# Last dense block: the last two F pieces taken by groups of 128 rows, each with its own signal, copy and store

## The chip, the cores and the metric

One core of a Trainium2 chip. The time of a kernel is the device time of one execution in microseconds (us); of several runs the median is given. The engines named below are PE (TensorE: the matmul stream, and PEld its weight loads), DVE (VectorE), ACT (ScalarE), POOL (GpSimd) and SP (SyncE, which here only issues DMAs). "L412" is line 412 of the kernel.

## What is computed

The program chains an attention-like recurrence, a routed mixture of experts, and a dense layer pair. Only the last part matters here; it works on x of 3072 rows and 384 columns:

```
def _moe2_ref(x, w_in, w_out):          # w_in 384 x 2048, w_out 2048 x 384
    h = x @ w_in
    relu6 = np.clip(h + 3.0, 0.0, 6.0)
    g = h * relu6 / 6.0
    return (g @ w_out).astype(np.float32)
```

Each product in fp32 is made of three matmuls in a faster format: every operand is split into a high and a low part, and hi·hi, hi·lo and lo·hi are added up in PSUM.

## The kernel before

**Tiling.** The dense part takes the 3072 rows in NBLK = 6 blocks of BLK = 512 rows. F2 = 2048 is cut into G2 = 16 pieces of 128. For each block and piece f, PE makes the piece of h, transposed (9 matmuls of 512 columns into one bank: 3 chunks of 128 of the 384 columns, 3 matmuls each); ACT makes `cut` from it (L692), DVE makes `g` (L1248), ACT rounds it to `g_hi` (L695), and DVE forms the rest `g_lo` (L1250), all on tiles of 128 x 512. The `g` tiles have F on the partitions and the 512 rows of the block along the free axis. Then the function `second` (L935) multiplies that piece by w_out: for each of the BT = 4 groups t of 128 rows, three matmuls of 384 columns (function `three`, L868 to L871) whose weights are the 128 columns t of `g_hi` and `g_lo`. They add into four banks `p_O[0..3]`, one for each group, which the trace calls bank_YT, bank_L, bank_P and bank_X. The first of the 16 pieces starts a bank's sum and the last ends it.

**Order on PE.** It is written out by hand in `blocks`. Piece f of h is followed by `second` of piece f - 2, so that the elementwise chain of a piece has time. After the loop over f come `second` of piece 14 and `second` of piece 15. In every block but the last, the next block's first pieces of h follow directly.

**The end of a block.** `second` of each piece adds 1 to the semaphore `s_O`. When it has counted all 16 pieces, ACT copies banks 0 and 1 to `o_sb` (L707) and adds 1 to `s_oA` after the second copy; DVE copies banks 2 and 3 (L1260) and adds 1 to `s_oV`. SP waits for `s_oA` and stores the first 256 rows (384 KB), then waits for `s_oV` and stores the other 256 rows (L410). The stores add 16 to `s_out[0]` and `s_out[1]`. At the very end SP waits for both (L417). The copies of a block wait for the stores of the block before, since `o_sb` has one buffer.

**Loops.** `dense_loop` writes blocks 0 and 1 out, runs blocks 2 and 3 as a hardware loop, and writes out blocks 4 and 5. Only block 5 has `last=True`. The input of block 5 is transposed during block 4, so SP has nothing but the two stores to do in block 5.

Of the kernel before, what the change touches and what calls it, by code (L numbers as in the profile page):

```python
# [9 lines left out]
ACT = mybir.ActivationFunctionType  # L10
AXX = mybir.AxisListType.X

P = 128
B, H, S, HD = 4, 8, 768, 48
D = H * HD
# [9 lines left out]
G2 = F2 // P  # L25
# [7 lines left out]
BLK = 512  # L33
NBLK = N // BLK
BT = BLK // P
# [2 lines left out]
TINY = 1e-9  # L38

ROUND = (4, 8, 12)  # L40
SHIFT = 4
RT_SHIFTED, RT_CHOICE, RT_SUMS, RT_TOTAL, RT_PICKED, RT_ALL = 3, 7, 8, 12, 13, 18
C_W1, C_W2 = (1, 2, 3), (1, 2, 3, 4)
# [27 lines left out]
def chained_moe_program(nc, r, k, v, w, u, w_skip, w_gate, w1, w2, w_in, w_out, out, x_dram, slot_dram):  # L71
    ctx = ExitStack()
    with ctx:
# [36 lines left out]
        p_mT, p_H, p_O = bank[0], bank[1:4], bank[4:8]  # L110
# [50 lines left out]
        wo_hi = sb("wo_hi", [P, G2, D], F32R)  # L161
# [13 lines left out]
        wo_lo = sb("wo_lo", [P, G2, D], F32R)  # L175
# [7 lines left out]
        class Region:  # L183
# [61 lines left out]
        g_hi = [de(f"g_hi{i}", [P, BLK], F32R) for i in range(4)]  # L245
        g_lo = [de(f"g_lo{i}", [P, BLK], F32R) for i in range(4)]
        o_sb = de("o_sb", [P, BT, D])
# [23 lines left out]
        s_m, s_mT, s_mhi, s_mlo, s_H, s_cut, s_g, s_ghi, s_glo, s_O, s_oA, s_oV = (  # L271
            sem(x) for x in ("s_m", "s_mT", "s_mhi", "s_mlo", "s_H", "s_cut", "s_g", "s_ghi", "s_glo", "s_O", "s_oA", "s_oV"))
        s_out = [sem(f"s_out{half}") for half in range(2)]
# [42 lines left out]
        def _(eng):  # L316
# [82 lines left out]
            def load_m(blk):  # L399
                eng.dma_start(m_in[:, :, :], x_dram[bass.ds(blk * BLK, BLK), :].rearrange("(t p) n -> p t n", p=P)).then_inc(s_m, 16)  # L400

            def blocks(blk, i, first=False, last=False):
                if not last:
                    if not first:
                        eng.wait_ge(s_mT, KC * blk + KC)
                    load_m(blk + 1)
                for half, done in enumerate((s_oA, s_oV)):
                    eng.wait_ge(done, blk + 2)
                    ts = slice(half * BT // 2, (half + 1) * BT // 2)
                    eng.dma_start(out[bass.ds(blk * BLK + half * (BLK // 2), BLK // 2), :].rearrange("(t p) n -> p t n", p=P),  # L410
                                  o_sb[:, ts, :]).then_inc(s_out[half], 16)
# [2 lines left out]
                eng.sem_inc(done, 16)  # L414
            dense_loop(eng, blocks)
            for done in s_out:
                eng.wait_ge(done, 16 * (NBLK + 1))  # L417


        @block.gpsimd  # L420
# [141 lines left out]
        def _(eng):  # L562
# [82 lines left out]
            def win_hi(f):  # L645

                piece = slice(f * P, (f + 1) * P)
                eng.activation(wi_hi[:, :, piece], wi_raw[:, :, piece], ACT.Copy).then_inc(s_wihi, 1)
# [37 lines left out]
            def blocks(blk, i, first=False, last=False):  # L686
                for f in range(G2):
                    t = G2 * blk + f
                    eng.wait_ge(s_H, t + 1)

                    eng.wait_ge(s_g, t + SHIFT - 1)
                    eng.activation(cut[f % 2][:, :], p_H[f % 3][:, :], ACT.Relu, bias=0.5, scale=1.0 / 6.0).then_inc(s_cut, 1)  # L692
                    eng.wait_ge(s_g, t + SHIFT + 1)
                    eng.wait_ge(s_O, t + SHIFT - 3)
                    eng.activation(g_hi[f % 4][:, :], g[f % 2][:, :], ACT.Copy).then_inc(s_ghi, 1)  # L695
                    if not last and f in ROUND:
                        rows_hi(1 - i, ROUND.index(f), KC * (blk + 1) + ROUND.index(f))
                    if first:
                        if f == 0:
                            eng.wait_ge(s_wo, 16 * W_PARTS)  # L700
                        wout_hi(f)
                        if f + HI_FIRST < G2:
                            win_hi(f + HI_FIRST)
                eng.wait_ge(s_O, G2 * (blk + 1) + SHIFT)
                eng.wait_ge(s_out[0], 16 * blk + 16)
                for t in range(BT // 2):
                    a = eng.activation(o_sb[:, t, :], p_O[t][:, 0:D], ACT.Copy)  # L707
                a.then_inc(s_oA, 1)
# [14 lines left out]
        def _(eng):  # L723
# [5 lines left out]
            for q in range(NPAIR):  # L729
                last = eng.transpose(p_X[:, q * P:(q + 1) * P], u_less[:, q:q + 1].to_broadcast([P, P]), ident[:, :])  # L730
            last.then_inc(s_uT, 1)
            eng.wait_ge(s_tab, TAB_K)
            for q in range(NPAIR):
                last = eng.transpose(p_kT[:, q * P:(q + 1) * P], powT_k[:, q, :], ident[:, :])
# [133 lines left out]
            def three(dst, a_hi, a_lo, b_hi, b_lo, start, stop):  # L868
                eng.matmul(dst, a_hi, b_hi, start=start, stop=False)  # L869
                eng.matmul(dst, a_hi, b_lo, start=False, stop=False)  # L870
                return eng.matmul(dst, a_lo, b_hi, start=False, stop=stop)  # L871
# [57 lines left out]
            def rows_mT(kc, done):  # L929
# [2 lines left out]
                    a = eng.transpose(p_mT[:, t * P:(t + 1) * P], m_in[:, t, kc * P:(kc + 1) * P], ident[:, :])  # L932
                a.then_inc(s_mT, 1)

            def second(blk, f, first=False):  # L935
                t0 = G2 * blk + f
                eng.wait_ge(s_glo, t0 + 1)
                if first:
                    eng.wait_ge(s_wolo, f + 1)
                if f == 0:  # L940
                    eng.wait_ge(s_oA, blk + 1)
                    eng.wait_ge(s_oV, blk + 1)
                for t in range(BT):
                    tok = slice(t * P, (t + 1) * P)
                    a = three(p_O[t][:, 0:D], g_hi[f % 4][:, tok], g_lo[f % 4][:, tok], wo_hi[:, f, :], wo_lo[:, f, :],
                              f == 0, f == G2 - 1)
                a.then_inc(s_O, 1)

            def blocks(blk, i, first=False, last=False):
                if not first:  # L950
                    eng.wait_ge(s_mlo, KC * (blk + 1))
                for f in range(G2):

                    eng.wait_ge(s_g, G2 * blk + (f - 1 if f < 2 else f - 2) + SHIFT)
                    if first:
                        eng.wait_ge(s_wilo, f + 1)
                    for kc in range(KC):
                        if first and f == 0:
                            eng.wait_ge(s_mlo, kc + 1)
                        piece = slice(f * P, (f + 1) * P)  # L960
                        a = three(p_H[f % 3][:, :], wi_hi[:, kc, piece], wi_lo[:, kc, piece],
                                  mT_hi[i][:, kc, :], mT_lo[i][:, kc, :], kc == 0, kc == KC - 1)
                    a.then_inc(s_H, 1)
                    if not last and f in ROUND:
                        kc = ROUND.index(f)
                        if kc == 0:
                            eng.wait_ge(s_m, 16 * (blk + 1))
                        rows_mT(kc, KC * (blk + 1) + kc)
                    if f >= 2:
                        second(blk, f - 2, first)  # L970
                second(blk, G2 - 2, first)
                second(blk, G2 - 1, first)

# [2 lines left out]
            for kc in range(KC):  # L976
                for t in range(TH):
                    for gain, done in ((gain_hi, s_gain_hi), (gain_lo, s_gain_lo)):
                        eng.wait_ge(done, t + 1)
                        a = eng.matmul(p_first_mT[kc], gain[t][:, kc * P:(kc + 1) * P], goes_to[t][:, :], start=False,  # L980
                                       stop=gain is gain_lo and t == TH - 1, skip_group_check=True)
# [5 lines left out]
        def _(eng):  # L987
            done = [0]
# [171 lines left out]
            last = NC - 1  # L1160
# [25 lines left out]
            def win_lo(f):  # L1186

                piece = slice(f * P, (f + 1) * P)
                eng.wait_ge(s_wihi, f + 1)
                eng.tensor_tensor(wi_lo[:, :, piece], wi_raw[:, :, piece], wi_hi[:, :, piece].bitcast(F32), ALU.subtract).then_inc(s_wilo, 1)  # L1190
# [52 lines left out]
            def blocks(blk, i, first=False, last=False):  # L1243
                for f in range(G2):
                    t = G2 * blk + f
                    eng.wait_ge(s_cut, t + 1)

                    eng.scalar_tensor_tensor(g[f % 2][:, :], cut[f % 2][:, :], 1.0, p_H[f % 3][:, :], ALU.min, ALU.mult).then_inc(s_g, 1)  # L1248
                    eng.wait_ge(s_ghi, t + 1)
                    eng.tensor_tensor(g_lo[f % 4][:, :], g[f % 2][:, :], g_hi[f % 4][:, :].bitcast(F32), ALU.subtract).then_inc(s_glo, 1)  # L1250
                    if not last and f in ROUND:
                        rows_lo(1 - i, ROUND.index(f), KC * (blk + 1) + ROUND.index(f))
                    if first:
                        wout_lo(f)
                        if f + LO_FIRST < G2:
                            win_lo(f + LO_FIRST)
                eng.wait_ge(s_O, G2 * (blk + 1) + SHIFT)
                eng.wait_ge(s_out[1], 16 * blk + 16)
                for t in range(BT // 2, BT):
                    a = eng.tensor_copy(o_sb[:, t, :], p_O[t][:, 0:D])  # L1260
                a.then_inc(s_oV, 1)
# [37 lines left out]
```

## Time and profile before

| | us |
|---|---|
| median of 3 runs (743.0 to 743.84) | 743.3 |
| the profiled execution, its own time | 737.41 |
| its span in the trace | 735.6 |
| PE busy in the span | 700.2 (95%) |
| end of the last matmul in the trace | 730.7 |

The span is what the instructions cover. The profiled execution's own time is 1.8 us longer than its span, and 5.9 us shorter than the median of the plain runs; differences within the trace are carried over to the median as they are. Matmul ends in the trace are modelled and overlap; the distance between the starts of two neighbours is the time that one takes in a stream.

### The profile page before, as it was taken

Reading aid. Unit: us, or ns where it says so; the run is one execution under the profiler, and the core shown is the slowest. Engines: PE = TensorE matmul, PEld = TensorE weight load, DVE = VectorE, ACT = ScalarE, POOL = GpSimd, SP = SyncE. Lnnn points to the kernel's source line nnn. Section 1 sums busy time; section 2 is a strip of 40 time slices with the busy share of each in tenths; the row PEclk is TensorE's granted clock in tenths of the full one; section 3 lists DMA queues with packets and bytes.
Section 4 is the critical chain, followed back from the end, with each engine's and each line's share of the span. In section 5 each row is a group of like instructions: output and inputs, shape, how many; then the busy total and the mean of one; then the engine's idle time right before and its main releaser. Section 6 shows DMA issues by size and latency. Waiting matters only on the chain.

```text
span 735.6 us, 13594 instructions
## 1 busy us (share of the span) xinstructions
PE 700.2 (95%) x5103; PEld 639.5 (87%) x5103; DVE 383.7 (52%) x767; ACT 324.3 (44%) x703; POOL 141.0 (19%) x189
## 2 busy tenths in 40 slices
PE   5999999929899999989999999999999999999997
PEld 3888888819899999979899899899999999998896
DVE  5576667566678888656544333433333333333332
ACT  3767767625555555635343232333233233223232
POOL 8648866450222222100000000000000000000000
PEclk9999999968999999999999999999999999999999
DMA  9788886114946666810002000200200020001001
GB/s 156 145 185 176 194 173 133 55 40 155 382 145 212 210 219 214 267 60 1 1 1 86 1 1 1 86 1 1 63 24 1 1 86 1 1 1 43 1 1 43
DMA packets 106986, 65.57 MB, mean 89 GB/s; under 512 B 79938, under 2 KB 102756, under 8 KB 106928
## 3 DMA queue, kind: packets, MB, share of 16 engines
q1 hardware_dynamic: 102864, 60.18, 30.6%
q0 software_dynamic: 2816, 4.60, 2.0%
q8 instruction: 37, 0.61, 0.3%
q10 hardware_dynamic: 1248, 0.02, 0.1%
q14 instruction: 21, 0.17, 0.1%
HBM read 53.69 MB, written 12.80 MB: 90 GB/s over the span
## 4 chain that ended last, share of the span: by engine, by line
PE 90%; DVE 2%; DMA 2%; ACT 2%; issue 2%; POOL 1%; POOLq 0%; DVEq 0%; SPq 0%; ACTq 0%
PE bank_A L870 8%; PE bank_A L871 8%; PE bank_A L869 8%; PE bank_A L807 4%; PE bank_L L869 4%; PE bank_L L871 4%; PE bank_L L870 4%; PE bank_P L871 4%; PE bank_P L870 4%; PE bank_P L869 4%; PE bank_kT L870 3%; PE bank_kT L871 3%; PE bank_kT L869 3%; PE bank_YT L871 3%; PE bank_YT L870 3%; PE bank_YT L869 3%
## 5 line engine op out<-in xcount | busy, mean ns | idle before, releaser
L1250 DVE TENSOR_TENSOR g_lo<-g,g_hi 128x512 fp32r<-128x512 f32 x96 | 66.5, 692 | 67.0 <-ACT g_hi L695 67.0
L695 ACT ACTIVATE g_hi<-g 128x512 fp32r<-128x512 f32 x96 | 60.7, 632 | 73.1 <-DVE g L1248 73.1
L1248 DVE SCALAR_TENSOR_TENSOR g<-cut,bank_A 128x512 f32<-128x512 f32 x60 | 41.2, 687 | 92.8 <-ACT cut L692 92.8
L692 ACT ACTIVATE cut<-bank_A 128x512 f32<-128x512 f32 x60 | 35.9, 598 | 101.3 <-PE bank_A L871 100.8
L871 PE MATMUL bank_A<-mT_hi,wi_lo 128*128 128x512 f32 x180 | 71.0, 394 | 0.0
L870 PE MATMUL bank_A<-mT_lo,wi_hi 128*128 128x512 f32 x180 | 70.9, 394 | 0.0
L869 PE MATMUL bank_A<-mT_hi,wi_hi 128*128 128x512 f32 x180 | 70.0, 389 | 0.0
L590 ACT ACTIVATE bank_A<-ident,own 128x128 f32<-128x128 f32 x192 | 59.1, 359 | 5.5 <-DVE A_sb L1041 3.0
L1248 DVE SCALAR_TENSOR_TENSOR g<-cut,bank_kT 128x512 f32<-128x512 f32 x36 | 24.7, 687 | 66.6 <-ACT cut L692 66.6
L692 ACT ACTIVATE cut<-bank_kT 128x512 f32<-128x512 f32 x36 | 21.5, 598 | 69.7 <-PE bank_kT L871 69.7
L674 ACT ACTIVATE hT_hi<-bank_A 128x256 fp32r<-128x256 f32 x48 | 18.4, 384 | 56.9 <-PE bank_A L871 56.9
L869 PE MATMUL bank_A<-xgT_hi,w_hi 128*128 128x256 f32 x144 | 41.6, 289 | 1.3 <-DVE xgT_lo L1207 1.3
L871 PE MATMUL bank_kT<-mT_hi,wi_lo 128*128 128x512 f32 x108 | 42.7, 396 | 0.0
L870 PE MATMUL bank_kT<-mT_lo,wi_hi 128*128 128x512 f32 x108 | 42.6, 395 | 0.0
L869 PE MATMUL bank_kT<-mT_hi,wi_hi 128*128 128x512 f32 x108 | 42.1, 390 | 0.1
L871 PE MATMUL bank_A<-xgT_hi,w_lo 128*128 128x256 f32 x144 | 41.5, 288 | 0.0
L870 PE MATMUL bank_A<-xgT_lo,w_hi 128*128 128x256 f32 x144 | 41.5, 288 | 0.0
L871 PEld LDWEIGHTS bank_A<-mT_hi,wi_lo 128*128 128x128 f32 x180 | 33.8, 188 | 7.2
L1041 DVE TENSOR_TENSOR A_sb<-bank_A,upto 128x512 f32<-128x512 f32 x48 | 30.9, 686 | 17.4 <-PE bank_A L807 17.2
L870 PEld LDWEIGHTS bank_A<-mT_lo,wi_hi 128*128 128x128 f32 x180 | 33.7, 187 | 6.0
L869 PEld LDWEIGHTS bank_A<-mT_hi,wi_hi 128*128 128x128 f32 x180 | 33.8, 188 | 5.7
L1218 DVE TENSOR_TENSOR w_lo<-raw,w_hi 128x384 fp32r<-128x384 f32 x64 | 35.9, 561 | 0.0
(240 smaller groups left out, 1848.3 us busy)
## 6 DMA issues: line engine op xcount, KB each, us to landing
raw<-in_moe_w_dram SPq DMA_DIRECT2D x24, 512.0 KB, 5.8
raw<-in_moe_w_dram SPq DMA_DIRECT2D x7, 1536.0 KB, 6.9
r_in<-in_r_dram SPq DMA_DIRECT2D x24, 192.0 KB, 4.4
k_in<-in_k_dram SPq DMA_DIRECT2D x24, 192.0 KB, 4.7
v_in<-in_v_dram SPq DMA_DIRECT2D x24, 192.0 KB, 3.4
x_scratch<-y_sb SPq DMA_DIRECT2D x24, 192.0 KB, 2.3
out_dram<-o_sb SPq DMA_DIRECT2D x12, 384.0 KB, 2.8
m_in<-x_scratch SPq DMA_DIRECT2D x5, 768.0 KB, 5.3
```

The costliest lines, as they stand in the source:

```text
L590: a = eng.activation(p_A[:, o, q * P:(q + 1) * P], ident[:, :], ACT.Copy, scale=own[n % 2][:, 2 * q + o:2 * q + o + 1])
L674: eng.activation(hT_hi[:, f, :], p_h[f % 3][:, 0:TT], ACT.Relu).then_inc(s_hhi, 1)
L692: eng.activation(cut[f % 2][:, :], p_H[f % 3][:, :], ACT.Relu, bias=0.5, scale=1.0 / 6.0).then_inc(s_cut, 1)
L695: eng.activation(g_hi[f % 4][:, :], g[f % 2][:, :], ACT.Copy).then_inc(s_ghi, 1)
L807: m = eng.matmul(p_A[:, o, q * P:(q + 1) * P], kT[i][half, q, :], rT[i][half, q, :], start=False, stop=True, skip_group_check=True)
L869: eng.matmul(dst, a_hi, b_hi, start=start, stop=False)
L870: eng.matmul(dst, a_hi, b_lo, start=False, stop=False)
L871: return eng.matmul(dst, a_lo, b_hi, start=False, stop=stop)
L1041: eng.tensor_tensor(A_sb[i][:, o, :, :], p_A[:, o, :].rearrange("s (q t) -> s q t", q=NPAIR), mask, ALU.mult).then_inc(s_Aev, 1)
L1218: eng.tensor_tensor(w2_lo[:, f, :], raw2[:, f, :], w2_hi[:, f, :].bitcast(F32), ALU.subtract).then_inc(s_w2lo, 1)
L1248: eng.scalar_tensor_tensor(g[f % 2][:, :], cut[f % 2][:, :], 1.0, p_H[f % 3][:, :], ALU.min, ALU.mult).then_inc(s_g, 1)
L1250: eng.tensor_tensor(g_lo[f % 4][:, :], g[f % 2][:, :], g_hi[f % 4][:, :].bitcast(F32), ALU.subtract).then_inc(s_glo, 1)
```

## The change

In the last block only, the order on PE after the loop over f is turned inside out: for each group t in the order 0, 2, 1, 3 first the three matmuls of piece 14 and then the three of piece 15, and then a signal. Each group is copied as soon as its signal is there, ACT taking groups 0 and 1 and DVE groups 2 and 3, each copy with its own count, and SP stores each group of 128 rows (192 KB) by itself, in the same order. The final wait counts two stores more in all, one for each of the two semaphores. In all blocks ACT and DVE now wait for the store of the block before ahead of the wait for `s_O`, and not behind it.

```
+LAST_ROWS = (0, 2, 1, 3)
...
 SP:
+                if last:
+                    for t in LAST_ROWS:
+                        half = t // (BT // 2)
+                        eng.wait_ge((s_oA, s_oV)[half], blk + 2 + t % (BT // 2))
+                        eng.dma_start(out[blk * BLK + t * P:blk * BLK + (t + 1) * P, :], o_sb[:, t, :]).then_inc(s_out[half], 16)
+                    return
...
-                eng.wait_ge(done, 16 * (NBLK + 1))
+                eng.wait_ge(done, 16 * (NBLK + BT // 2))
...
 ACT:
+                eng.wait_ge(s_out[0], 16 * blk + 16)
+                if last:
+                    for t in range(BT // 2):
+                        eng.wait_ge(s_O, G2 * blk + G2 - 2 + SHIFT + LAST_ROWS.index(t) + 1)
+                        eng.activation(o_sb[:, t, :], p_O[t][:, 0:D], ACT.Copy).then_inc(s_oA, 1)
+                    return
                 eng.wait_ge(s_O, G2 * (blk + 1) + SHIFT)
-                eng.wait_ge(s_out[0], 16 * blk + 16)
...
 PE:
+            def product(t, f):
+
+                tok = slice(t * P, (t + 1) * P)
+                return three(p_O[t][:, 0:D], g_hi[f % 4][:, tok], g_lo[f % 4][:, tok], wo_hi[:, f, :], wo_lo[:, f, :],
+                             f == 0, f == G2 - 1)
...
                 for t in range(BT):
-                    tok = slice(t * P, (t + 1) * P)
-                    a = three(p_O[t][:, 0:D], g_hi[f % 4][:, tok], g_lo[f % 4][:, tok], wo_hi[:, f, :], wo_lo[:, f, :],
-                              f == 0, f == G2 - 1)
+                    a = product(t, f)
                 a.then_inc(s_O, 1)
...
+                if last:
+                    for t in LAST_ROWS:
+                        for f in (G2 - 2, G2 - 1):
+                            eng.wait_ge(s_glo, G2 * blk + f + 1)
+                            a = product(t, f)
+                        a.then_inc(s_O, 1)
+                    return
                 second(blk, G2 - 2, first)
                 second(blk, G2 - 1, first)
...
 DVE:
+                eng.wait_ge(s_out[1], 16 * blk + 16)
+                if last:
+                    for t in range(BT // 2, BT):
+                        eng.wait_ge(s_O, G2 * blk + G2 - 2 + SHIFT + LAST_ROWS.index(t) + 1)
+                        eng.tensor_copy(o_sb[:, t, :], p_O[t][:, 0:D]).then_inc(s_oV, 1)
+                    return
                 eng.wait_ge(s_O, G2 * (blk + 1) + SHIFT)
-                eng.wait_ge(s_out[1], 16 * blk + 16)
```

## Rows read from the trace of the kernel before

**Rows 1.** The page: PE busy and its clock in 40 slices; the chain by engine
```profile
PE   5999999929899999989999999999999999999997
...
PEclk9999999968999999999999999999999999999999
...
PE 90%; DVE 2%; DMA 2%; ACT 2%; issue 2%; POOL 1%; POOLq 0%; DVEq 0%; SPq 0%; ACTq 0%
```

**Rows 2.** Timeline, 730.3 to 736 us: start, duration, engine, line, what
```profile
730.36 0.34 PE L871 MATMUL bank_X<-wo_hi,g_lo 128*128 128x384 f32 x1
730.73 0.49 ACT L707 ACTIVATE o_sb<-bank_YT 128x384 f32<-128x384 f32 x1 [4.28 <-PE bank_X L871]
730.73 0.56 DVE L1260 COPY o_sb<-bank_P 128x384 f32<-128x384 f32 x1 [3.56 <-PE bank_X L871]
731.12 0.48 ACT L707 ACTIVATE o_sb<-bank_L 128x384 f32<-128x384 f32 x1
731.21 0.55 DVE L1260 COPY o_sb<-bank_X 128x384 f32<-128x384 f32 x1
731.63 0.89 SPq L410 DMA_DIRECT2D out_dram<-o_sb  x2
```

**Rows 3.** Stores and SP's waits at the end: duration ns min/median/max, landing counted from issue
```profile
L410 SPq DMA_DIRECT2D out_dram<-o_sb x2: 372/420/469, 731.6 to 732.0; - x2
...
DMA to landing us min/median/max: 2.5/2.8/3.1
...
SPq L417 <- DMA out_dram<-o_sb: 2.6, 1, 2.6
...
L73 SPq COMPARE_BRANCH  x1: 38/38/38, 735.2 to 735.2; - x1
```

**Rows 4.** Windows at the end: stretch, length, busy of PE, PEld, DVE, ACT, POOL, clock, DMA share, GB/s
```profile
731.63:732.52 0.89, 0.00 (x0) 0.00 (x0) 0.12 (x1) 0.00 (x0) 0.00 (x0) 1.00 0.01 2
732.52:734.70 2.18, 0.00 (x0) 0.00 (x0) 0.00 (x0) 0.00 (x0) 0.00 (x0) 1.00 1.01 359
734.70:735.60 0.90, 0.00 (x0) 0.00 (x0) 0.00 (x0) 0.00 (x0) 0.00 (x0) 0.82 0.01 3
```

**Rows 5.** Timeline, 726.2 to 728.5 us: `second` of piece 14 starts, g_lo of piece 15
```profile
726.37 0.33 PE L869 MATMUL bank_YT<-wo_hi,g_hi 128*128 128x384 f32 x1
726.48 0.69 DVE L1250 TENSOR_TENSOR g_lo<-g,g_hi 128x512 fp32r<-128x512 f32 x1 [0.70 <-ACT g_hi L695]
...
726.72 0.33 PE L871 MATMUL bank_YT<-wo_hi,g_lo 128*128 128x384 f32 x1
...
726.89 0.33 PE L869 MATMUL bank_L<-wo_hi,g_hi 128*128 128x384 f32 x1
...
728.45 0.33 PE L869 MATMUL bank_YT<-wo_hi,g_hi 128*128 128x384 f32 x1
```

**Rows 6.** Timeline, 322.5 to 326 us: a short wait of PE for DVE
```profile
323.63 0.69 DVE L1241 TENSOR_TENSOR mT_lo<-bank_X,mT_hi 128x512 fp32r<-128x512 f32 x1 [0.52 <-ACT mT_hi L684]
...
323.94 0.39 PE L871 MATMUL bank_kT<-mT_hi,wi_lo 128*128 128x512 f32 x1
...
324.38 0.19 PEld L869 LDWEIGHTS bank_kT<-mT_hi,wi_hi 128*128 128x128 f32 x1 [0.48 <-DVE mT_lo L1241]
324.38 0.50 PE L869 MATMUL bank_kT<-mT_hi,wi_hi 128*128 128x512 f32 x1
324.49 0.19 PEld L870 LDWEIGHTS bank_kT<-mT_lo,wi_hi 128*128 128x128 f32 x1
324.72 0.40 PE L870 MATMUL bank_kT<-mT_lo,wi_hi 128*128 128x512 f32 x1
```

**Rows 7.** The copies to o_sb in all six blocks: count, duration ns min/median/max
```profile
L1260 DVE COPY o_sb<-bank_P x6: 557/558/558, 391.4 to 730.7; 128x384 f32<-128x384 f32 x6
L1260 DVE COPY o_sb<-bank_X x6: 547/547/548, 391.9 to 731.2; 128x384 f32<-128x384 f32 x6
```

**Rows 8.** Stores of 192 KB in the first part: all 24; that of 150.3; that of 145.2
```profile
x_scratch<-y_sb SPq DMA_DIRECT2D x24, 192.0 KB, 2.3
...
L326 SPq DMA_DIRECT2D x_scratch<-y_sb x1: 320/320/320, 150.3 to 150.3; - x1
...
DMA to landing us min/median/max: 1.9/1.9/1.9
...
L326 SPq DMA_DIRECT2D x_scratch<-y_sb x1: 319/319/319, 145.2 to 145.2; - x1
...
DMA to landing us min/median/max: 2.5/2.5/2.5
```

**Rows 9.** Windows around PE's idle time ahead of the dense part
```profile
316.00:318.40 2.40, 0.06 (x2) 0.03 (x1) 2.34 (x5) 0.49 (x2) 0.97 (x1) 1.00 0.13 45
...
319.00:321.00 2.00, 2.00 (x6) 1.63 (x5) 0.36 (x2) 0.60 (x1) 0.00 (x0) 0.50 0.40 57
...
324.00:326.00 2.00, 1.95 (x9) 1.36 (x8) 1.26 (x3) 0.60 (x1) 0.00 (x0) 1.00 0.00 0
```

## The prediction, made before the changed kernel ran

> **What bounds the kernel now.** I read the page's slices first: PE is busy nine tenths of nearly every slice, falls in the very last one, and makes 90% of the chain of waits [rows 1]. The change touches nothing that PE does before 726 us, so the question is only how long the tail is behind the last matmuls. The timeline of the end comes next. The last matmul starts at 730.36; 0.37 later ACT and DVE both start copying, two banks each; ACT is done at 731.60, DVE at 731.76 [rows 2]. SP issues the first store at 731.63, right behind ACT, and the second at 732.05: the two issues fill 0.89 us to 732.52, and the second is the one of 0.47 [rows 2, 3]. The windows show data moving from 732.52 to 734.70 at 359 GB/s with all DMA engines busy: 0.79 MB cannot go faster [rows 4]. The stores land 2.5 and 3.1 us after their issue, so the last at 732.05 + 3.1 = 735.15, which agrees with SP's wait of 2.6 us from 732.52 on and its branch at 735.2; the span ends at 735.6, 0.45 later [rows 3]. From the last matmul's start to the end are thus 5.2 us, with nothing for PE to do. Two parts of them hang on the amount of work: the second copy of each engine, and 2.2 us of transfer, since all of the block's output starts at once.
>
> **The change part by part.**
>
> PE issues the same 24 matmuls of 384 columns. In a stream they are 0.174 us apart (726.37 to 728.45 for twelve) [rows 5]; six a group are 1.04 us. Only the order differs, with eight waits on `s_glo` where there were two. Now the three matmuls of group 0, piece 15, come fourth, in the slot of 726.89, and not at 728.45. They need `g_lo` of piece 15, which DVE ends at 726.48 + 0.69 = 727.17 [rows 5]. So **a new stall** appears that was hidden by nine matmuls of piece 14. Its price by the nearest event: mT_lo ended at 324.32, the weight load began at 324.38 (0.06 later) and the next load at 324.49, which is when the first matmul really entered (0.11); the matmul after it started at 324.72 against 323.94 + 2 x 0.23 = 324.40, a loss of 0.32, the same as 324.49 against 324.17 [rows 6]. Here that gives a load at 727.23, entry at 727.34, and a loss of 727.34 - 726.89 = **+0.45 us**. Bounds: at least 727.17 - 726.89 = 0.28; at most, were the whole load of 0.19 exposed, 727.42 - 726.89 = 0.53. Queued behind this wait are the 21 remaining matmuls; all move by 0.45. The other waits on `s_glo` are met by then: nothing. The last matmul starts at 730.81, not 730.36.
>
> Copies. By the same 0.37 behind a group's last matmul, groups 0, 2, 1 and 3 can be copied from 728.06, 729.10, 730.14 and 731.18. Each engine gets one every 2.1 us and needs 0.49 (ACT) or 0.56, so the first three lie beside PE's work. Would a copy be slower while PE writes other banks? In the five earlier blocks the copies ran beside PE and took 547 to 558 ns, as in the last [rows 7]. Behind PE remains one DVE copy of 0.55: done at 731.73. Only 0.03 is won on the old 731.76, since the stall eats nearly what the dropped copy gives.
>
> Stores. SP has two DMAs more, four of 0.32 to 0.47 each, about 1.04 apart, in the order in which the groups come; nothing waits behind them on SP, POOL issues nothing here. The third is issued near 730.66 and its 196 KB are through by 732.1. The fourth is issued at 731.76 (0.03 behind the copy, as before): 732.05 - 731.76 = **-0.29 us**, because it no longer stands behind a neighbour's issue. Its landing is the term that decides. In this profile 24 stores have just this form (128 partitions x 384 fp32 to DRAM): the median of 2.3 is taken among other traffic, the one at 150.3 on a quiet machine took 1.9 and the worst that I count as quiet (145.2) took 2.5 [rows 8]. The last store will be alone, so I take 1.95, nearest to the 1.9: landing at 733.71. Against 3.1 that is **-1.15 us**; at 2.5 it would be -0.6. The windows agree: 0.20 MB at 359 GB/s are 0.55 us, a quarter of the 2.2 that pass now.
>
> On the size of the DMA the Trainium skill speaks against the change: "DMA: Bandwidth & Descriptors", section "Rules for kernel authors", says to put small transfers together, and its anatomy section gives each DMA a fixed 2.0 us plus bytes over 436 GB/s, measured on the GpSimd path. By that 192 KB would take 2.45, an estimate from the page, and the gain would be 0.5 less; the 1.9 of [rows 8] says otherwise.
>
> The waits on `s_out` that moved ahead of `s_O` ask for stores issued a block (68 us) earlier: nothing, either way. The end of the program behind the last landing stays 0.45, with one wait more that is already met.
>
> **Sum.** -0.29 - 1.15 = -1.44 (the +0.45 of PE and the -0.48 of the dropped copy are both in the -0.29). The profiled execution would take 737.41 - 1.44 = 735.97. It stands 5.9 us under the median of the runs, and nothing in the tail suggests that the change touches that offset: 743.3 - 1.4 = **741.9**. With both bounds at their good ends (stall 0.28, landing 1.9) the gain is 1.66, at their bad ends (0.53, 2.5) 0.81: 741.6 to 742.5.
>
> A measurement of this kernel can tell about 0.2%, which is 1.49 us, from no change. The forecast lies just short of it.
>
> **The rivals.**
>
> *A slower landing.* The last store takes 2.3 to 2.5, as the median and the quiet bad case of [rows 8] do, because starting a transfer and confirming it in DRAM does not shrink. Gain 0.9 to 1.1: 742.3. For it: one of the quiet stores did so. Against: the store at 150.3. The page's fixed cost points the same way. Chance 0.22.
>
> *Slower: the clock falls in the stall.* PE idles for about 0.45 us in front of its last 21 matmuls. After 2.4 us of idle time the granted clock of this kernel fell from 1.00 to 0.50, that is from 2.4 to 1.2 GHz, and matmuls ran so for over 3 us [rows 9]. If the new stall did that, the busy 21 x 0.174 = 3.65 us would at most double: +3.65 - 1.44 = +2.2, 745.5. It decides once more than 1.44 / 0.174, about 8 matmuls, run at the lower level. Against: the comparable wait of 0.44 us was followed by a window at 1.00 [rows 6, 9]. Chance 0.03.
>
> *The change doesn't do what it says, because the stores don't overlap.* If each had to land before the next starts moving, four of 1.95 from 728.6 on would end at 736.4, +1.2. Against: the two stores now, issued 0.42 apart, land 1.0 apart and not 2.5 [rows 3]. Chance 0.01.
>
> *No stall, or hardly one,* because matmuls of piece 14 get through later than the trace's starts say. Gain 1.7 and more: 741.5. The wait in [rows 6] speaks against it. Chance 0.06.
>
> *Nothing measurable is won,* because some engine's end that I don't see holds the program open. The last chain is stores, and SP's wait ends it [rows 3]. Chance 0.04.
>
> **How the numbers follow.** The forecast (gain 1.2 to 1.6) has 0.64. Since 1.44 lies 0.05 short of the bound of 1.49 and medians scatter by some 0.3, I give it a little less than half on the faster side: 0.30, plus 0.05 from the case without a stall and some 0.04 from scatter in the slow landing, 0.39. Slower by over 0.2% needs the clock or the stores in series: 0.04. The rest, 0.57, is within 0.2%. The range reaches from the case without a stall, with scatter (741.3), over the slow landing with scatter (742.9).
>
> **What would show it.** In the timeline of after: a gap on PE's weight loads from 726.9 to 727.2, ended by DVE's g_lo; 24 matmuls still 0.174 apart behind it; last matmul start near 730.8; copies 1.04 apart; four stores, the last near 731.76 and alone; landing 1.9 to 2.0; the span near 734.2. A gap over 0.6, a landing over 2.4, a clock under 1.00 in 727 to 731, or copies queued behind each other would prove the step in question wrong.

## The result, and the profile after

Over 22 runs each the changed kernel has a median of 742.11 us against 743.85 before. The recorded ratio, taken over all the runs, is 0.9979, with a 95% interval from 0.9969 to 0.9989 (the two medians alone give 0.9977). On the 743.3 us of the forecast that is 741.7, a gain of 1.56 us (0.8 to 2.3), where 741.9 and 1.44 were forecast. The gain lies at the bound of 0.2% that the forecast drew, a trifle beyond it. The interval covers both sides, so the side on which it falls is chance. Two stray executions of the later runs, one of 1762.7 us and one of 2070.15, are in no ratio.

The profiled execution of the changed kernel took 740.89 us with a span of 739.1, **longer** than the 737.41 and 735.6 of before. Single executions of either kernel differ by that much (740.2 to 745.5 in these runs), and the difference lies far from the change: the first matmul of the dense part starts at 322.8 before and at 327.8 after, while from there to the first product of piece 14 in block 5 both take 403.6 us, as do all the runs below. So the two traces are compared from that last point on. **The tail**, from the start of that matmul (bank_YT, `g_hi`) to the end of the span, is 735.6 - 726.37 = 9.23 us before [rows 5] and 739.1 - 731.37 = 7.73 after: 1.50 less. Spans have one decimal, so a tail is good to 0.05 and a difference of two to 0.1.

The timeline of after, 731.3 to 737 us (start, duration, engine, line, what), with the lines that answer to [rows 5] first:

```profile
731.37 0.33 PE L881 MATMUL bank_YT<-wo_hi,g_hi 128*128 128x384 f32 x1
731.48 0.69 DVE L1273 TENSOR_TENSOR g_lo<-g,g_hi 128x512 fp32r<-128x512 f32 x1 [0.70 <-ACT g_hi L702]
...
732.23 0.19 PEld L881 LDWEIGHTS bank_YT<-wo_hi,g_hi 128*128 128x128 f32 x1 [0.49 <-DVE g_lo L1273]
732.23 0.45 PE L881 MATMUL bank_YT<-wo_hi,g_hi 128*128 128x384 f32 x1 [0.17 <-DVE g_lo L1273]
732.34 0.19 PEld L882 LDWEIGHTS bank_YT<-wo_lo,g_hi 128*128 128x128 f32 x1
732.51 0.34 PE L882 MATMUL bank_YT<-wo_lo,g_hi 128*128 128x384 f32 x1
...
733.13 0.49 ACT L715 ACTIVATE o_sb<-bank_YT 128x384 f32<-128x384 f32 x1 [1.68 <-PE bank_YT L883]
...
733.65 3.48 SPq L412 DMA_DIRECT2D out_dram<-o_sb  x4
...
735.83 0.34 PE L883 MATMUL bank_X<-wo_hi,g_lo 128*128 128x384 f32 x1
736.21 0.56 DVE L1284 COPY o_sb<-bank_X 128x384 f32<-128x384 f32 x1 [1.46 <-PE bank_X L883]
```

The fourth matmul now waits for DVE: `g_lo` ends at 732.17, the weight load starts 0.06 later, and the next load at 732.34, when the first matmul has entered. In an unbroken stream it would have entered at 731.37 + 3 x 0.174 = 731.89: a stall of 0.45. The trace prints 0.49 for the load engine, counted from the end of its last load, and 0.17 for PE, since it counts a matmul as busy for 0.33 us while the next enters after 0.17; neither is the loss. The last matmul starts 4.46 us into the tail and not 3.99 [rows 2, 5]. One copy, DVE's, is behind it in place of two on each engine, and ends at 736.77. The window over the 21 matmuls behind the stall (length, busy of PE, PEld, DVE, ACT, POOL, granted clock, DMA share, GB/s) shows the clock at 1.00:

```profile
732.34:736.00 3.66, 3.66 (x21) 3.51 (x21) 0.56 (x1) 0.98 (x2) 0.00 (x0) 1.00 0.25 90
```

The stores of after, which answer to [rows 3] (duration ns, then landing us from issue, min/median/max), and SP's waits in the tail:

```profile
L412 SPq DMA_DIRECT2D out_dram<-o_sb x4: 332/338/345, 733.6 to 736.8; - x4
...
DMA to landing us min/median/max: 1.8/1.9/1.9
...
SPq L424 <- DMA out_dram<-o_sb: 1.5, 1, 1.5
...
L424 SPq EVENT_SEMAPHORE  x1: 17/17/17, 738.7 to 738.7; - x1
```

The DMA view of the last 4.0 us of each kernel, in slices of 0.1 us (busy tenths of the DMA engines, then GB/s), before from 731.6 on and then after from 735.1 on:

```profile
DMA  0000000007899999999999999999997100000000
GB/s 0 0 0 0 0 0 0 0 0 261 307 399 353 323 353 384 384 399 338 400 338 399 338 399 338 399 338 399 338 399 246 31 0 0 0 0 0 0 0 0
```

```profile
DMA  0000068989600078989500000699996100000000
GB/s 0 0 0 0 0 246 323 430 323 415 215 16 0 0 276 323 415 323 415 200 16 0 0 0 0 215 338 399 338 399 246 31 0 0 0 0 0 0 0 0
```

Before, one unbroken stretch of 2.2 us; after, short bursts of some 0.6 us that never touch, three of the four in view. Two of them come behind the start of the last matmul (735.83), at 736.5 and 737.6, and only the last lies behind the last copy as well. Behind the last burst, in both, come the same eight empty slices until the end.

### The profile page after: what moved, and what is told of

It reads as the page before. It is cut to its first block, busy times and chain, and to the rows that moved or that the text cites. A ratio compares the mean times of both kernels' runs of the same rounds, so it can differ in the third digit from the quotient of the medians.

```text
span 739.1 us, 13596 instructions
## 1 busy us (share of the span) xinstructions
PE 699.9 (95%) x5103; PEld 638.1 (86%) x5103; DVE 385.5 (52%) x767; ACT 324.4 (44%) x703; POOL 141.2 (19%) x189
## 4 chain that ended last, share of the span: by engine, by line
PE 86%; ACT 4%; DVE 3%; issue 3%; DMA 2%; another core or an unknown queue 1%; POOL 1%; POOLq 0%; ACTq 0%; SPq 0%; DVEq 0%
PE bank_A L882 8%; PE bank_A L883 8%; PE bank_A L881 8%; PE bank_A L819 4%; PE bank_L L881 4%; PE bank_L L883 4%; PE bank_L L882 4%; PE bank_P L883 4%; PE bank_P L882 4%; PE bank_P L881 4%; PE bank_kT L882 3%; PE bank_kT L883 3%; PE bank_kT L881 3%; PE bank_YT L883 3%; PE bank_YT L881 3%; PE bank_YT L882 3%
## 5 line engine op out<-in xcount | busy, mean ns | idle before, releaser
L819 PE MATMUL bank_A<-rT,kT 64*128 64x128 f32 x384 | 28.8, 290 | 8.8 <-ACT bank_A L597 6.1
```

The lines of the kernel that those rows point to most:

```text
L819: m = eng.matmul(p_A[:, o, q * P:(q + 1) * P], kT[i][half, q, :], rT[i][half, q, :], start=False, stop=True, skip_group_check=True)
```

## The experiments

Whole-kernel times scatter by some 0.5% between executions, so ratios have intervals of about 0.15% and can't part kernels that differ by half a us. The tails can. Here are both kernels and all twelve runs, with the tail read from the same anchor, the first matmul of piece 14's products. Where group 2 comes first, that is one into bank_P. Where piece 15 comes first, the anchor is put 0.11 before the start of DVE's `g_lo`; in the others it lies 0.11 to 0.12 before it.

| kernel | tail, us | ratio to before, 95% interval |
|---|---|---|
| before | 9.23 | 1 |
| the change | 7.73 | 0.9979 (0.9969 to 0.9989) |
| the change again (a0) | 7.77 | 0.9978 (0.9966 to 0.9990) |
| the change a third time (c1) | 7.78 | 0.9976 (0.9960 to 0.9992) |
| order 14, then 15, rest as the change (a1) | 7.37 | 0.9970 (0.9956 to 0.9984) |
| groups in pairs (a2) | 7.27 | 0.9979 (0.9963 to 0.9995) |
| pairs, ending on ACT (b3) | 7.09 | 0.9975 (0.9959 to 0.9991) |
| the same again (c2) | 7.16 | 0.9973 (0.9955 to 0.9992) |
| the same, final waits swapped (c4) | 7.20 | profile only |
| the change's order alone (a3) | 9.76 | 1.0010 (0.9996 to 1.0023) |
| two stores of 384 KB (b1) | 8.26 | 0.9999 (0.9982 to 1.0015) |
| copies only at the end (b2) | 9.28 | 1.0005 (0.9987 to 1.0024) |
| piece 15 of group 0 first (b4) | 8.24 | 0.9996 (0.9981 to 1.0010) |
| only the waits for old stores moved (c3) | 9.30 | 1.0000 (0.9984 to 1.0017) |

The ratios are the recorded ones and not quotients of medians (for a2 the medians would give 0.9993). Where a tail is 1 us shorter (b1, b4) they show no gain, and don't exclude it either. The tail of before stems from one profile, with c3 as its nearest repeat; that of the change was taken three times.

**The change again.**

> The changed kernel again. Tail = from the start of the first matmul of piece 14's products in the last block (bank_YT<-wo_hi,g_hi) to the end of the span: 9.23 us before, 7.73 us in the one profile of after. Theory (the gain is the last store, 192 KB alone in place of two of 384 KB, issued 0.3 us earlier in spite of a PE stall of 0.45 us): tail 7.7 to 7.8, time 1.5 us under before. Rival (the time differs because the earlier stages of the program ran otherwise): tail changes from profile to profile by more than 0.2 us.

> The changed kernel a third time, as the neighbour of the version below on one chip. Theory: tail 7.7 to 7.8, ratio to before 0.998. Rival (the ratio was luck of runs that scatter by 0.5% for other reasons): ratio 0.999 to 1.001 with the tail still 1.5 us shorter.

Tails of 7.77 and 7.78, ratios of 0.9978 and 0.9976. With spans as far apart as 732.3, 737.7 and 739.1 us, the tail moved by 0.05 in all, so the rival, a tail that moves by over 0.2, falls. The mean of the three is 7.76, so the change takes 1.47 us off the tail.

**PE's order alone.** In ACT's and DVE's branches for the last block and on SP:

```
-                        eng.wait_ge(s_O, G2 * blk + G2 - 2 + SHIFT + LAST_ROWS.index(t) + 1)
+                        eng.wait_ge(s_O, G2 * blk + G2 - 2 + SHIFT + BT)
...
-                    for t in LAST_ROWS:
-                        half = t // (BT // 2)
+                    for half, done in enumerate((s_oA, s_oV)):
+                        eng.wait_ge(done, blk + 3)
...
```

> PE's order of the change (group by group, stall included) alone; both engines copy only after the last group, and two stores of 384 KB as before. Theory: only the stall is left of the change: tail 9.23 + 0.45 = 9.7, time 0.4 to 0.5 us over before. Rival (the inside-out order itself brings something, for instance shorter matmul distances): tail 9.2 or less.

The tail is 9.76, 0.53 over before, where 0.45 was expected. The last matmul starts at 737.37 - 732.94 = 4.43 and not 3.99, which is the stall; another 0.06 is a later start of the copies (below), and the rest is within the rounding. The group-by-group order by itself brings nothing and costs its stall.

**No stall: two other orders on PE.** First, piece 14 of all groups and then piece 15 of all, with the signals, copies and stores of the change:

```
-                    for t in LAST_ROWS:
-                        for f in (G2 - 2, G2 - 1):
-                            eng.wait_ge(s_glo, G2 * blk + f + 1)
-                            a = product(t, f)
-                        a.then_inc(s_O, 1)
+                    for t, f in [(t, G2 - 2) for t in LAST_ROWS] + [(t, G2 - 1) for t in LAST_ROWS]:
+                        eng.wait_ge(s_glo, G2 * blk + f + 1)
+                        a = product(t, f)
+                        if f == G2 - 1:
+                            a.then_inc(s_O, 1)
```

> PE takes pieces 14 and 15 in the old sense (all groups of 14, then all of 15, groups in the order 0, 2, 1, 3); signals, copies and stores by group as in the change. No wait for g_lo, so the last matmul starts 3.99 us into the tail and not 4.46; groups end 0.52 apart and not 1.04. Theory: the PE stall is worth 0.45 us and the last store still lands in 1.9 to 2.0: tail 7.3, time 0.4 us under after. Rival (the reordering is what makes the gain, since it spaces the stores 1 us apart): the four stores, each 0.55 us of transfer, 0.52 us apart, run into each other, the last lands in 2.3 to 2.5: tail 7.6 to 7.8, no better than after.

The tail is 7.37, 0.39 under the change. The last matmul starts 736.22 - 732.23 = 3.99 into it. Its timeline and stores (as above):

```profile
736.22 0.34 PE L883 MATMUL bank_X<-wo_hi,g_lo 128*128 128x384 f32 x1
736.59 0.56 DVE L1284 COPY o_sb<-bank_X 128x384 f32<-128x384 f32 x1 [0.42 <-PE bank_X L883]
```

```profile
L412 SPq DMA_DIRECT2D out_dram<-o_sb x4: 344/351/453, 735.6 to 737.2; - x4
DMA to landing us min/median/max: 1.9/1.9/2.0
```

The stores come 0.52 us apart and move for 0.55 each, yet the slowest lands in 2.0. Crowding costs 0.1 of the 0.47 that the missing stall gives; the reordering is not what makes the gain.

Second, the groups in pairs, so that six matmuls cover the wait and the last two groups still end 1.04 apart:

```
+                    for t, f in ((0, G2 - 2), (2, G2 - 2), (0, G2 - 1), (2, G2 - 1), (1, G2 - 2), (1, G2 - 1), (3, G2 - 2), (3, G2 - 1)):
```

> As the change, but PE takes piece 14 of groups 0 and 2, then piece 15 of both, then groups 1 and 3 one after the other. Piece 15 is first needed 6 x 0.174 = 1.04 us into the tail, 0.1 to 0.2 us later than g_lo is done (0.80). Theory: no stall, stores of the last two groups still 1.04 us apart: last matmul starts at 3.99, tail 7.27 to 7.3, time 0.4 to 0.5 us under after. Rival (the stall costs nothing at the end because the last store's landing is bounded otherwise): tail 7.7.

Tail 7.27, as expected, and in its waits from 733.6 us on no line of PE or PEld is left:

```profile
ACT o_sb L715 <- PE bank_YT L883: 1.7, 1, 1.7
DVE o_sb L1284 <- PE bank_P L883: 1.5, 1, 1.5
DVE o_sb L1284 <- PE bank_X L883: 1.5, 1, 1.5
ACT o_sb L715 <- PE bank_L L883: 1.0, 1, 1.0
ACT g_hi L702 <- DVE g L1271: 0.8, 1, 0.8
DVE g_lo L1273 <- ACT g_hi L702: 0.7, 1, 0.7
```

**A longer stall.** For group 0, piece 15 comes before piece 14 (the matmul that ends the bank's sum is then piece 14's):

```
-                        for f in (G2 - 2, G2 - 1):
+                        for f in (G2 - 1, G2 - 2) if t == 0 else (G2 - 2, G2 - 1):
```

> The change, but for group 0 PE takes piece 15 before piece 14, so that the wait for g_lo comes with the very first product and the stall grows by 3 matmuls: from 0.45 to 0.45 + 0.52 = 0.97 us. Theory (every us of stall moves the end by a us, clock stays at full speed): tail 7.73 + 0.52 = 8.25, granted clock 1.00. Rival (a stall of PE ahead of its last 24 matmuls brings the clock down to half): matmuls 0.35 us apart, tail over 9.

Timeline, and the window over the last 24 matmuls (length, busy of PE, PEld, DVE, ACT, POOL, granted clock, DMA share, GB/s):

```profile
728.29 0.34 PE L883 MATMUL bank_X<-wo_hi,g_lo 128*128 128x384 f32 x1
728.57 0.69 DVE L1273 TENSOR_TENSOR g_lo<-g,g_hi 128x512 fp32r<-128x512 f32 x1 [0.70 <-ACT g_hi L702]
729.32 0.19 PEld L881 LDWEIGHTS bank_YT<-wo_hi,g_hi 128*128 128x128 f32 x1 [1.01 <-DVE g_lo L1273]
729.32 0.44 PE L881 MATMUL bank_YT<-wo_hi,g_hi 128*128 128x384 f32 x1 [0.69 <-DVE g_lo L1273]
...
729.60 0.34 PE L882 MATMUL bank_YT<-wo_lo,g_hi 128*128 128x384 f32 x1
```

```profile
729.00:733.80 4.80, 4.46 (x24) 4.14 (x24) 0.82 (x2) 0.98 (x2) 0.00 (x0) 1.00 0.23 81
```

The entry at 729.43 comes 0.97 after the stream's slot of 728.46, and the tail is 8.24, 0.48 over the change's mean for 0.52 more stall. A stall in front of the last products moves the end by its own length. The clock stayed at 1.00 (2.4 GHz) even behind this twice as long gap.

**The size of the last store.** Order and copies as in the change, but two stores as before (SP's edit of the run with PE's order alone):

> The change with two stores of 384 KB (groups 0 and 1 after ACT's second copy, groups 2 and 3 after DVE's second) in place of four of 192 KB; order and copies as in the change. The last store is issued at the same time as in after, but is twice as large, and the first still moves when it starts. Theory (the size of what still has to move at the end decides): landing 2.5, tail 7.73 + 0.6 = 8.3. Rival (what counts is that copies and stores start early; a store costs a fixed time): tail 7.7 to 7.9.

```profile
L412 SPq DMA_DIRECT2D out_dram<-o_sb x2: 372/372/373, 732.6 to 733.7; - x2
...
DMA to landing us min/median/max: 2.5/2.5/2.5
```

The tail is 8.26, 0.50 over the mean of the change. The last store starts at the same point behind the last copy and lands in 2.5 and not 1.9. So of the 1.47 some 0.5 are the size of the stores, and the other 0.97 come from starting the copies and the first half of the output earlier, net of the stall.

**Small stores, late copies.** Four stores of 192 KB, with all copies behind the last group's signal (ACT's and DVE's edit of the run with PE's order alone):

> The change with four stores of 192 KB, but all copies wait for the last group's signal. The transfers then form one stretch of 2.2 us behind the copies. Theory (0.79 MB at 359 GB/s, started 0.4 us earlier than with stores by halves, plus the stall of 0.45): tail 9.2 to 9.4. Rival (small stores land fast however they come): last store issued near 6.4 us into the tail, lands in 1.9, tail 8.8.

```profile
DMA to landing us min/median/max: 1.9/2.1/2.1
```

The tail is 9.28. The single stores land almost as quickly as alone, but the last is issued late: four issues of 345 to 462 ns in a row take 1.82 us on SP, and the DMA view of this run shows the data moving in one unbroken stretch of 2.2 us, as before. That stretch starts earlier, since the first store is issued 5.39 us into the tail and not 5.76 as in a3. Cutting the stores without spreading them gains, against the 9.76 of PE's order alone, 0.48, just the stall's price.

The four kernels with the change's order on PE, and thus the same stall, can be set side by side. Early copies and stores take off 1.50 with two large stores (9.76 to 8.26) and 1.52 with four small ones (9.28 to 7.76), 0.06 of each being the later start of the copies (below); small stores take off 0.48 with late copies and 0.50 with early ones. The two parts simply add up, and spreading is three times as large.

**The moved waits alone.** The kernel before with `wait_ge(s_out[..])` ahead of `wait_ge(s_O, ..)` on ACT and DVE:

> The kernel before, with nothing but the waits for the earlier block's store moved ahead of the waits for the last product. Theory: those stores landed some 60 us earlier, nothing changes: tail 9.2, ratio 1.000. Rival (with the semaphore of PE waited for last, the copies start sooner, or with one more hop later): copies start other than 0.37 us behind the last matmul's start, tail off by 0.05 or more.

```profile
731.29 0.34 PE L871 MATMUL bank_X<-wo_hi,g_lo 128*128 128x384 f32 x1
731.72 0.49 ACT L707 ACTIVATE o_sb<-bank_YT 128x384 f32<-128x384 f32 x1 [4.34 <-PE bank_X L871]
731.73 0.56 DVE L1260 COPY o_sb<-bank_P 128x384 f32<-128x384 f32 x1 [3.63 <-PE bank_X L871]
```

The rival holds here: the copies start 0.43 behind the last matmul's start, against 0.37 before [rows 2], and the tail is 9.30. The runs a3 and b2, which have the moved waits too, show the same 0.43. The move is not free: it costs 0.06 us where the end hangs on it. In the change only each engine's first copy pays (733.13 is 0.44 behind its matmul, at 732.69); the last one starts 0.38 behind its own. Why the order of two waits matters when one of them has long been met was not tried further.

**A version that is better than both.** Pairs, and an order that ends on ACT, whose copy is shorter:

```
-LAST_ROWS = (0, 2, 1, 3)
+LAST_ROWS = (2, 0, 3, 1)
...
+                    for t, f in ((2, G2 - 2), (0, G2 - 2), (2, G2 - 1), (0, G2 - 1), (3, G2 - 2), (3, G2 - 1), (1, G2 - 2), (1, G2 - 1)):
```

> Groups in the order 2, 0, 3, 1, in pairs (2 and 0 share piece 14, then piece 15; then 3, then 1), so that the last copy is ACT's, 0.49 us in place of DVE's 0.56. Theory: as the order in pairs that ends on DVE (tail 7.3) less 0.06: 7.2 to 7.25. Rival (ACT's copy is signalled later than DVE's): no less than 7.3.

> Groups in pairs, ending on ACT's copy, again, beside the changed kernel. Theory: tail 7.1 to 7.2, 0.6 us under the changed kernel and 2.1 us under before, ratio to before 0.997. Rival (tail of 7.1 was a chance of one profile): tail 7.3.

> Pairs ending on ACT, with the two final waits of SP in the other order in the source. In the trace the semaphore wait comes at the landing of group 3 and the branch behind it at the landing of group 1; in the changed kernel the semaphore wait itself ended last. Theory (ending on the branch saves one instruction behind the last landing): with the order swapped tail 7.2 in place of 7.1. Rival (the 0.1 us came from ACT's copy and rounding of the span): tail 7.1 as before.

Tails of 7.09 and 7.16: 0.6 under the change, 2.1 under before. Beside the changed kernel on the same chip the ratios are 0.9973 and 0.9976, which their intervals can't part; that it is faster rests on the tails. ACT's copy gives 0.07 of the step from 7.27. The swap of the final waits gave 7.20: the sign is the expected one, but 0.04 to 0.11 on spans of one decimal settles nothing.

## Why the prediction was right, step by step

*The stall of 0.45.* Right to the printed digit: a load 0.06 behind `g_lo`, an entry 0.11 behind the load, as read from [rows 6]. The runs without it (a1, a2) and with twice of it (b4) gave -0.39, -0.49 and +0.48 in the tail.

*PE's stream of 0.174.* Nearly: the matmuls right behind the stall came up to 0.18 apart, so the last one starts 0.47 later and not 0.45 (0.44 to 0.47 in the repeats and the other runs with this stall).

*Copies.* Right: 736.77 is 5.40 into the tail; the forecast's 731.73 was 5.36. The copies of the first three groups cost nothing.

*The store.* The forecast took 1.95 for its landing from the quiet store of [rows 8] and set the 2.5 aside; it measured 1.8 to 1.9 in all four stores, and 1.9 in the repeats. The last was issued at 733.65 + 3.48 - 0.34 = 736.79, 5.42 into the tail, against 5.68 before: -0.26 for the forecast's -0.29. The landing then gives -1.2. By b1, half of that is the size: there 384 KB, issued 1.12 behind their neighbour and not 0.42, took 2.5 and not 3.1. The end of the program behind the landing came to 0.41 for 0.45, within the rounding. So the sum fits to 0.03 partly because small misses in both directions cancel. The slow-landing rival falls. So does what the Trainium skill makes of this size ("DMA: Bandwidth & Descriptors", the anatomy of one DMA): its 2.45, an estimate from a fit on the GpSimd path, is about 0.55 over what these stores from SP took.

*The waits on `s_out`, costed at nothing.* Wrong in principle, by 0.06 us where a block's end is exposed; it did not touch the sum, since the last copy escapes it. That it does was luck: the forecast gave the move no cost at all.

*The other rivals.* The stall is there, and the end of the program is SP's wait for the last store, so neither the case without a stall nor that of an unseen end holds. The clock stayed at 1.00 behind gaps of 0.45 and 0.97. The stores did not wait for one another; in the change they never overlap, and where they do (a1, b2) the slowest lands in 2.0 to 2.1.

*The span near 734.2.* This sign failed: the profiled execution had 739.1, and the spans of the change in three profiles are 732.3, 737.7 and 739.1. A difference within one trace does not give the span of another; here only the tail could be forecast, and the absolute 741.9 rests on a base (743.3, of three runs) that the 22 runs put at 743.85.

The sum came to 1.47 in the tail for 1.44, and to 1.56 (0.8 to 2.3) by the ratio. What the forecast left on the table is that the same signals with a better order of PE's products would have given 0.5 more in the tail.

## What to carry to other kernels

At the end of a program count what must still happen behind the last matmul: one copy, one issue, one transfer. Cut the last unit of output small, and spread the earlier ones over the time in which the matmuls still run; here the spreading was worth 1.5 us and the small stores 0.5, and small stores that all started at the end still moved in one stretch as long as before. When products are regrouped to finish one group early, ask which operand is now needed sooner, and put as many independent matmuls in front of it as its wait is long.

## What the runs showed of the hardware that was not expected

- Two waits ahead of an instruction are not symmetric: with the one that is met last in second place, ACT's and DVE's copies started 0.43 us behind the last matmul's start, in first place 0.37.
- Four stores of 192 KB, 0.52 us apart and each 0.55 us of transfer (an estimate: 0.20 MB at 359 GB/s), cost only 0.1 us in the last landing over stores 1.04 apart.
- The scatter between executions comes from what runs ahead of the dense part. Its first matmul starts between 320.96 and 330.06 us in the fourteen profiles, and from there to the anchor it is 403.6 in each. A share of that comes from the recurrence: most of its steps, seen by the stores to x_scratch, take 5.20 us, but every fourth step from the seventh on takes 6.21 in some executions and up to 7.31 in others of the same instructions (before: 77.59 to 83.80; after: 79.63 to 86.84). The change does not decide it: the changed kernel has the long steps in two profiles and 6.21 in the third (c1). All of a0 to a3 have long ones, all of the b and c runs only the short. What does decide was not looked into.

SP's DMA issues around that step, of before and then of after:

```profile
77.59 0.34 SPq L326 DMA_DIRECT2D x_scratch<-y_sb  x1
...
83.80 0.34 SPq L326 DMA_DIRECT2D x_scratch<-y_sb  x1
```

```profile
79.63 0.34 SPq L327 DMA_DIRECT2D x_scratch<-y_sb  x1
...
86.84 0.34 SPq L327 DMA_DIRECT2D x_scratch<-y_sb  x1
```
